# The first tile of a fused attention and two-layer kernel, cut into two units of 256 columns, with a new order for the first chunk

## The reference

```python
for t in range(S):
    kt, vt, bt = (k_n[:, :, t], v[:, :, t], beta[:, :, t, None])
    y[:, :, t] = np.einsum('bhd,bhde->bhe', q[:, :, t], state)
    v_old = np.einsum('bhde,bhd->bhe', state, kt)
    state = state + bt[:, :, :, None] * np.einsum('bhd,bhe->bhde', kt, vt - v_old)
...
h = x @ w_in                                         # layer 1, [384, 2048]
g = np.maximum(h, 0.0) + np.log1p(np.exp(-np.abs(h)))
x = g @ w_out                                        # [2048, 384]
h = x @ moe2_w_in;  g = h * np.cos(h);  out = g @ moe2_w_out
```

## Time and profile before

| | |
|---|---|
| three runs | 1145.91, 1149.58, 1151.12 us; median 1149.58 |
| profiled execution | 1146.16 us |
| its span | 1144.4 us |
| TensorE busy | 1026.4 us (90%) |
| VectorE, ScalarE, GpSimd busy | 747.3, 504.4, 328.0 us |

### The profile page before, as it was taken

One profiled execution on the slowest core, in us unless ns is written; L12 is line 12 of the kernel. 1 busy time (PEld: TensorE's weight loads), 2 busy tenths in 40 slices (PEclk: granted clock), 3 DMA queues, 4 the chain that ended last, 5 costly groups with the idle time before them and its releaser, 6 DMA issues.

```text
span 1144.4 us, 24969 instructions
## 1 busy us (share of the span) xinstructions
PE 1026.4 (90%) x10904; PEld 870.3 (76%) x10904; DVE 747.3 (65%) x1081; ACT 504.4 (44%) x802; POOL 328.0 (29%) x376
## 2 busy tenths in 40 slices
PE   3047779998999899899999999999999999999997
PEld 2046657876887787677778878889999999999996
DVE  4985444674567475837554468787777768777775
ACT  4131334355344634453463354454454545445443
POOL 3171850393069009602930017520010101001000
PEclk9556679999999999999989999999999999999999
DMA  9121301211030102011010071110202002010101
GB/s 206 49 70 30 43 1 30 47 12 43 16 57 29 28 18 43 29 29 23 9 43 16 2 221 35 60 45 1 56 1 56 1 1 56 1 28 1 29 1 28
DMA packets 101212, 42.69 MB, mean 37 GB/s; under 512 B 77008, under 2 KB 96464, under 8 KB 101104
## 3 DMA queue, kind: packets, MB, share of 16 engines
q1 hardware_dynamic: 100160, 40.90, 16.2%
q10 hardware_dynamic: 944, 0.20, 0.1%
HBM read 31.65 MB, written 9.44 MB: 36 GB/s over the span
## 4 chain that ended last, share of the span: by engine, by line
PE 63%; POOL 19%; DVE 11%; issue 4%; ACT 2%; DMA 0%; SPq 0%; DVEq 0%; ACTq 0%
POOL inv L378 10%; PE bank L1122 9%; PE bank L1124 9%; PE bank L1123 8%; POOL blk L375 8%; PE bank L1142 6%; PE bank L1144 6%; PE bank L1143 6%; DVE blk L654 3%; PE bank L1146 3%; PE bank L1148 3%; PE bank L1147 3%; PE bank L897 2%; PE bank L885 2%; PE bank L955 1%
## 5 line engine op out<-in xcount | busy, mean ns | idle before, releaser
L1122 PE MATMUL bank<-x_hi,wi_hi 128*128 128x512 f32 x576 | 236.9, 411 | 1.3 <-DVE x_lo L689 1.3
L1124 PE MATMUL bank<-x_hi,wi_lo 128*128 128x512 f32 x576 | 230.1, 399 | 0.0
L1123 PE MATMUL bank<-x_lo,wi_hi 128*128 128x512 f32 x576 | 229.5, 398 | 0.0
L580 ACT ACTIVATE tmp<-bank 128x512 f32<-128x512 f32 x96 | 57.5, 599 | 260.2 <-PE bank L1124 260.1
L839 DVE TENSOR_TENSOR g_lo<-tmp,g_hi 128x512 fp32r<-128x512 f32 x192 | 162.5, 847 | 6.6
L830 DVE SCALAR_TENSOR_TENSOR tmp<-bank,tmp 128x512 f32<-128x512 f32 x96 | 65.9, 686 | 153.7 <-ACT tmp L584 153.3
L571 ACT ACTIVATE tmp<-bank,consts 128x512 f32<-128x512 f32 x96 | 66.1, 689 | 177.2 <-PE bank L1124 177.2
L1142 PE MATMUL bank<-wo_hi,g_hi 128*128 128x384 f32 x384 | 129.5, 337 | 1.8 <-DVE g_lo L839 1.8
L1124 PEld LDWEIGHTS bank<-x_hi,wi_lo 128*128 128x128 f32 x576 | 110.2, 191 | 26.9
L1144 PE MATMUL bank<-wo_hi,g_lo 128*128 128x384 f32 x384 | 129.4, 337 | 0.0
L1143 PE MATMUL bank<-wo_lo,g_hi 128*128 128x384 f32 x384 | 129.1, 336 | 0.0
(11 more groups left out here) (100 smaller groups left out, 1572.0 us busy)
## 6 DMA issues: line engine op xcount, KB each, us to landing
stage<-in_moe_w_in SPq DMA_DIRECT2D x32, 192.0 KB, 4.4
stage<-in_moe_w_out SPq DMA_DIRECT2D x8, 768.0 KB, 5.6
kn<-in_k SPq DMA_DIRECT2D x24, 192.0 KB, 4.5
res_v<-in_v SPq DMA_DIRECT2D x24, 192.0 KB, 3.8
qn<-in_q SPq DMA_DIRECT2D x24, 192.0 KB, 4.4
x_t<-x_res SPq DMA_DIRECT2D x6, 768.0 KB, 4.2
x_raw<-x_t SPq DMA_DIRECT2D x6, 768.0 KB, 6.1
out_x<-res SPq DMA_DIRECT2D x24, 192.0 KB, 3.2
```

What stands on the lines that cost most here:

```text
L1122: mm(dst, wi_hi[:, ft, kt, :], hi[:, kt, :], start=(kt == 0), stop=False)
L1123: mm(dst, wi_hi[:, ft, kt, :], lo[:, kt, :], start=False, stop=False)
L1124: last = mm(dst, wi_lo[:, ft, kt, :], hi[:, kt, :], start=False, stop=(kt == KT - 1))
```

## The change

The first tile becomes two units of 256 columns: columns 0 to 255 are the first 64 tokens of the four batches, and need YT0 only. So there are 13 units (2, then 5 tiles of layer 1, then 6 of layer 2), and the first product is issued behind YT0 of chunk 0. In detail:

- Chunk 0's first half is written out in `begin` in an order of its own: the keys of chunk 1 are transposed and the scores P0 are computed ahead of the first substitution's end. What is left of chunk 0 (17 jobs) goes beside unit 0, chunk 1 beside unit 1, chunk c beside tile c-1.
- SLOTS is replaced by AT: for each unit the slots at which a job is issued. The first four jobs in the rows of units 2 to 5 belong to the chunk before (norms of a later chunk).
- The first substitution writes its products densely into `delta`, instead of into the unused half of `blk` with a stride.
- The norms' factors use three rows in place of four; chunk 1's keys are scaled by GpSimd. Two of the four diagonal copies of chunk 0 go to VectorE. Half of the first keys are loaded on ScalarE's queue, and the beta blocks on SP's; q and v of chunk 0 are loaded earlier; the last weight piece is loaded behind v.
- Six weight pieces instead of seven are split early by ScalarE and GpSimd; GpSimd starts the fourth once invT is set, not once `inv` is ready.

```diff
-LAST = 2 * TILES * FT
-FUSED = (TILES - 1) * FT
+
+HALF = NT // 2
+UNITS = [(0, 0, HALF), (0, HALF, HALF)] + [(t, 0, NT) for t in range(1, TILES)] + [(t, 0, NT) for t in range(TILES)]
+N1 = TILES + 1
+NU = len(UNITS)
+LAST1 = N1 * FT
+LAST = NU * FT
+FUSED = (N1 - 1) * FT
...
-FRONT = ("T0", "T1", "S0", "S1")
-ORDER = ("KS0", "M1", "Q0", "F1", "P0", "T0", "V0", "T1", "SN0", "S0", "S1", "Y0", "KS1", "V1", "YT0", "SN1",
+BEGIN = ("T0", "T1", "S0", "S1", "Q0", "P0", "+T0", "+T1", "M1", "F1", "V0", "SN0", "Y0", "YT0")
+FIRST = ("KS1", "+S0", "+S1", "V1", "Q1", "SN1", "P1", "Y1", "YT1")
+ORDER = ("KS0", "M1", "Q0", "F1", "P0", "+T0", "V0", "+T1", "SN0", "+S0", "+S1", "Y0", "KS1", "V1", "YT0", "SN1",
          "Q1", "P1", "Y1", "YT1")
...
+AT = (
+    (0, 1, 2, 3, 4, 5, 6, 7, 8, 9, 11, 12, 14, 18, 19, 20, 21),
+    (3, 7, 8, 10, 11, 12, 13, 14, 15, 16, 17, 18, 19, 20, 20, 21, 21, 22, 23, 24, 24, 25, 26, 27, 28, 29),
+    (0, 1, 2, 3, 4, 10, 11, 12, 13, 14, 15, 15, 16, 17, 18, 19, 20, 21, 21, 22, 22, 23, 24, 24, 25, 26, 27, 27, 28, 29),
...
+def jobs_at(i, slot):
+    return AT[i].count(slot)
...
         load_k(0)
         for n in range(2):
             load_piece(stage1, w1_loaded, pieces1, n)
         load_k(1)
-        for n in range(2, RING):
+        load_q(0)
+        load_piece(stage1, w1_loaded, pieces1, 2)
+        load_beta_blocks()
+        load_piece(stage1, w1_loaded, pieces1, 3)
+        load_v(0)
+        for n in range(RING, RING + 2):
+            sp.wait_ge(w_split, piece_before(n) + 1)
             load_piece(stage1, w1_loaded, pieces1, n)
-        load_v(0)
-        load_q(0)
-        for n in range(RING, NP):
+        sp.wait_ge(filled, cid(0, "Q0") + 2)
+        load_q(1)
+        for n in range(RING + 2, NP - 1):
             sp.wait_ge(w_split, piece_before(n) + 1)
             load_piece(stage1, w1_loaded, pieces1, n)
...
+        def scale_keys(c):
+            pool.wait_ge(norm_step, 6 * c + 6)
+            g = 2 * c % 4
+            keys = kn[:, g:g + 2, :, 0:D]
+            nc.gpsimd.tensor_tensor(keys, keys, norm[:, 2, :].rearrange("p (s u) -> p s u", s=2).unsqueeze(3)
+                                    .to_broadcast([P, 2, U, D]), ALU.mult).then_inc(kn_set, 1)
+
         clean(0)
-        for n in range(RING):
+        for n in range(2):
             low_weights(n)
-        pool.wait_ge(inv_ready, 1)
-        for n in range(RING, EARLY):
+        scale_keys(1)
+        low_weights(2)
+        pool.wait_ge(invT_set, 1)
+        for n in range(3, EARLY):
             low_weights(n)
         for n in range(EARLY, NP):
...
+        for s in range(2):
+            src = k[2:4].rearrange("b h s d -> s (b h) d")[s * C:(s + 1) * C, :, :]
+            nc.scalar.dma_start(kn[C:P, s, :, 0:D], src).then_inc(k_loaded[0], 16)
+        nc.scalar.dma_start(beta_rows[:, :], beta.rearrange("b h s -> (b h) s")).then_inc(beta_loaded, 16)
...
-            for n in range(RING):
+            for n in range(2):
                 high_weights(n)
+            take_transposes(0, "Q0", qT)
+            high_weights(2)
+            take_transposes(1, "T0", knT[:, fill_of(1, 0)])
+            take_transposes(1, "T1", knT[:, fill_of(1, 1)])
+            for n in range(3, EARLY):
+                high_weights(n)
+            fill_diagonal(0, (1, 0))
+            act.wait_ge(diag_set, 4)
+            take_merge(0, "M1", BLK, lambda part, s: m1[part, s], 1.0)
+            take_merge(0, "F1", 0, lambda part, s: aT[part, fill_of(0, s), :, BLK:C], -1.0)
+            take_y(0, "Y0")
+            take_x(0, 0, "YT0")
 
...
             for j in range(BLK - 1):
-                prod = blk[:, 0:j + 1, j + 1:BLK].rearrange("p c i -> p i c")
                 shape = [P, BLK - 1 - j, j + 1]
+                prod = flat(delta[:, :, :])[:, 0:shape[1] * shape[2]].rearrange("p (i c) -> p i c", c=shape[2])
...
             take_s(0, 0, "S0")
+            factors(1)
             take_s(0, 1, "S1")
             for g in range(4):
                 take_blocks(0, g)
+            take_p(0, "P0")
             first_solve()
+            turn_inverse(0)
+            dve.wait_ge(w_split, 3)
+            transpose_inverse(0)
+            dve.wait_ge(invT_set, 1)
+            for g in (3, 2):
+                rows, lo = slice(BLK * g, BLK * g + BLK), BLK * (g % 2)
+                nc.vector.tensor_copy(aT[rows, both(0), :, lo:lo + BLK],
+                                      invT[rows, :, :].rearrange("p (s u) c -> p s u c", s=2)).then_inc(diag_set, 1)
+            take_delta(0, 0, "V0")
+            take_state(0, 0, "SN0")
+            take_x(0, 0, "YT0")
 
...
                 gram(0, s)
+            pe.wait_ge(q_loaded, 32)
+            transposes(0, "Q0", qn)
+            scores(0, 0)
+            for s in range(2):
+                keys_transposed(1, s)
+            merge_inner(0)
+            merge_outer(0)
+            solve_values(0, 0, "V0")
+            add_to_state(0, 0, "SN0")
+            read_out(0, 0, "Y0")
+            turn_out(0, "YT0", "Y0")
 
...
+            t, at, w = UNITS[i]
+            if i in (0, N1):
+                await_weights(part_of(i), True, ft)
             if ft == 0:
-                if t < TILES:
-                    await_pair(pe, cid(t, "YT1"))
+                if i < N1:
+                    await_pair(pe, cid(t, "YT1" if i else "YT0"))
                 else:
-                    pe.wait_ge(x_lo_set, t - TILES + 1)
+                    pe.wait_ge(x_lo_set, t + 1)
             if before(n) is not None:
                 pe.wait_ge(h_used, before(n) + 1)
             hi, lo = x_hi[t % 2], x_lo[t % 2]
-            dst = bank[4 + ring(n)][:, :]
+            dst, cols = bank[4 + ring(n)][:, 0:w], slice(at, at + w)
             for kt in range(KT):
-                mm(dst, wi_hi[:, ft, kt, :], hi[:, kt, :], start=(kt == 0), stop=False)
-                mm(dst, wi_hi[:, ft, kt, :], lo[:, kt, :], start=False, stop=False)
-                last = mm(dst, wi_lo[:, ft, kt, :], hi[:, kt, :], start=False, stop=(kt == KT - 1))
+                mm(dst, wi_hi[:, ft, kt, :], hi[:, kt, cols], start=(kt == 0), stop=False)
+                mm(dst, wi_hi[:, ft, kt, :], lo[:, kt, cols], start=False, stop=False)
+                last = mm(dst, wi_lo[:, ft, kt, :], hi[:, kt, cols], start=False, stop=(kt == KT - 1))
...
         begin()
         jobs = attention()
-        for _ in range(JOBS):
-            next(jobs)
         product1(0)
-        for t in range(TILES - 1):
+        for i in range(N1 - 1):
             for ft in range(FT):
-                n = t * FT + ft
+                n = i * FT + ft
                 product1(n + 1)
-                for _ in range(SLOTS[2 * ft]):
+                for _ in range(jobs_at(i, 2 * ft)):
                     next(jobs)
                 product2(n)
-                for _ in range(SLOTS[2 * ft + 1]):
+                for _ in range(jobs_at(i, 2 * ft + 1)):
                     next(jobs)
...
```

More of the change, by code:

```diff
@@ L122, in build @@
         beta_blk = sb("beta_blk", [P, NCH, BLK], where=att)
-        norm = sb("norm", [P, 4, 2 * U], where=att)
+        norm = sb("norm", [P, 3, 2 * U], where=att)
         kn = sb("kn", [P, 4, U, Q2], where=att)
@@ L319, in _ @@
             load_piece(stage2, w2_loaded, pieces2, n)
-        store_x2(TILES - 2)
-        for t in (TILES, TILES + 1):
+        store_x2(N1 - 2)
+        for t in range(2):
             load_x(t)
@@ L418, in _ @@
             if n == 3:
-                low_x(TILES)
-        for t in range(TILES + 1, 2 * TILES):
+                low_x(0)
+        for t in range(1, TILES):
             low_x(t)
@@ L455, in take_merge, with fill_diagonal @@
                 last.then_inc(taken[n % 3], 1)
-        def fill_diagonal(c):
+        def fill_diagonal(c, groups):
             act.wait_ge(invT_set, c + 1)
-            for g in range(4):
+            for g in groups:
                 rows, lo = slice(BLK * g, BLK * g + BLK), BLK * (g % 2)
@@ new lines, in begin @@
+            take_delta(0, 0, "V0")
+            take_state(0, 0, "SN0")
+            take_x(0, 0, "YT0")
+        def attention():
+            take_rest(0, 1, "KS1")
+            yield
+            take_s(1, 0, "S0")
+            yield
+            take_s(1, 1, "S1")
+            yield
+            take_delta(0, 1, "V1")
+            yield
+            take_blocks(1, 0)
+            yield
+            yield
+            take_state(0, 1, "SN1")
+            yield
+            take_blocks(1, 1)
+            yield
+            take_p(0, "P1")
+            yield
+            take_blocks(1, 2)
+            yield
+            yield
+            take_blocks(1, 3)
+            yield
+            take_x(0, 1, "YT1")
+            yield
+            yield
+            reduce(2)
+            yield
+            yield
+            factors(2)
+            scale_keys(2)
+            yield
+            for c in range(1, NCH):
@@ L1039, in begin @@
                 gram(0, s)
-        def attention():
```

(39 more changed lines are left out.)

291 lines of the change are left out of this document (156 added, 135 removed), and 3 rows, old and new, of the table AT.

## The result

The changed kernel takes 1171.21 us (median of 4 runs, 1166.83 to 1173.26) against 1149.25 for the kernel before in the same pairs of runs: a ratio of 1.0187, 95% interval 1.0165 to 1.0208. It is **slower by 1.9%**, clear of noise, and outside the range of the prediction (1130 to 1159). The profiled execution took 1172.83 us.

The account below looks back on a forecast made before the run. GpSimd's substitution and the stretch from a merge to the next substitution were taken to bound the kernel. Chunk 2's substitution +1.8 us and 4.2 less behind the last merge gave -2.4: 1147 us, range 1130 to 1159.

Parts of the forecast that it names:

- Part 1: Road to the first product: copy of the merge's result at 69.6 plus 20.5 us, product at 90 instead of 131.5.
- keys loaded on two queues: Start of the front: half of the first keys on ScalarE's queue, taken to save 1.5 us.
- the dense products don't help: Rival on the first substitution: dense writing saves nothing, front 7.2 us later, +4.8, 1154 us; chance 0.10.
- Part 2: First product to chunk 1's substitution: 32.5 us, so start at 122.6 (113.75 before), merge at 175.4.
- the weight loads: Rival: weight loads bound the 256-column matmuls, 0.174 us or so each instead of 0.12, 1158 us; chance 0.15.
- it waits 8: Merge of chunk 1: TensorE could be there at about 167, merge at 175.4, so it waits 8 us.
- the ring doesn't bind: Rival: the early start is kept, less moved chunk-0 jobs and some 10 us for 256-column products, -16, 1133; chance 0.20.
- the ring: GpSimd's substitution, merge, then the stretch to the next substitution: 106.2 us per 512-token tile, taken to set the time.
- Part 3: Chunk 1's merge to chunk 2's substitution: 43.1 us instead of 53.5, so start at 218.5, 1.8 us later than before.
- Part 4: From chunk 2's substitution on: old periods kept, 4.2 us less behind the last merge, total -2.4 us.
- The sign: Whole kernel against before: chance 0.34 faster, 0.41 the same, 0.25 slower.
- the price of the split: First tile as two 256-column halves: +2 us over both units in the forecast, some 10 us in a rival.

Follow-up runs that it names:

- e5_early: Changed kernel's front and dense products, first tile whole, old slots, chunk 1's gram products and block transposes moved into the front; 1130.25 us, 0.983 of the kernel before.
- e1_odd: Changed kernel with steps from the merge (chunk 1) or the inverse's turn (chunks 2 to 4) one slot earlier, merges at odd slots; 1158.86 us, ratio 1.0068.
- e6_split: Changed kernel's front, first tile as two 256-column units, both begun after 128 tokens, slots of e1_odd from the second unit; 1167.71 us, ratio 1.0148.
- e10_halves: e5_early with its first tile as two 256-column units, both begun after 128 tokens, steps at nearly the same share of the tile; 1151.12 us, ratio 1.0008.
- e2_shift: Kernel before with all steps from the inverse's turn on one slot later, nothing else; 1181.87 us, ratio 1.0273.

## Why the prediction was wrong

**Part 1 was right.** Predicted: first product at 90, steps of 255 elements at 0.42 us, one of two VectorE copies over 3 us (they took 0.69 and 3.80). The timeline has

```profile
50.00 0.42 DVE L803 TENSOR_TENSOR delta<-blk,inv 128x255 f32<-128x255 f32 x1
...
66.33 4.52 DVE L841 COPY aT<-invT 32x1024 f32<-32x1024 f32 x2
...
66.37 3.93 POOL L427 TENSOR_TENSOR wi_lo<-stage,wi_hi 128x1536 fp32r<-128x1536 f32 x1 [33.26 <-DVE invT L820]
...
70.89 1.19 ACT L477 ACTIVATE m<-bank 32x512 f32<-32x512 f32 x2 [2.42 <-DVE aT L841]
...
92.10 0.55 PE L1284 MATMUL bank<-x_hi,wi_hi 128*128 128x256 f32 x1 [1.40 <-DVE x_lo L762]
```

The copy of `m` was due at 69.6 and came at 70.89; the product came at 92.10. A term that did not come is the 1.5 us for keys loaded on two queues: the squares start at 9.11 us, and at 8.86 in the kernel before, and the multiply ahead of the steps at 36.59 instead of 35.0. The dense steps fell from 0.59 to 0.42 us, and those of 31 elements stayed at 0.19 to 0.21, so a further element costs about 1.0 ns (0.22 us over 224 elements) where it cost 1.7: the rule of the Trainium skill named there (Vector Engine (DVE) Microarchitecture Reference, section 5.2) holds, and the rival "the dense products don't help" is out.

**Part 2 was right in its sum, and that by luck in part.** Predicted 122.6 for the substitution of chunk 1, measured 122.80: the first product was 2.1 us late, and the stretch behind it took 30.7 us for 32.5 (whose listed jobs add up to 14.9, not 14.7). Its inverse was turned after 46.5 us instead of 49.3, so the merge came at 172.85 for 175.4. The matmuls of 256 columns at full clock stand 0.12 us apart, as taken:

```profile
117.64 0.28 PE L1310 MATMUL bank<-g_lo,wo_hi 128*128 128x256 f32 x1
117.76 0.28 PE L1311 MATMUL bank<-g_hi,wo_lo 128*128 128x256 f32 x1
```

against 512 columns in e5_early

```profile
226.45 0.40 PE L1307 MATMUL bank<-g_hi,wo_lo 128*128 128x512 f32 x1
226.69 0.39 PE L1305 MATMUL bank<-g_hi,wo_hi 128*128 128x512 f32 x1
```

So the weight loads bound neither, and that rival fell. But "it waits 8" at that merge was wrong: TensorE waited 0.9, because it had already lost 10.1 us to waits for g_lo since 92. I had named this uncovered chain in the rival where the ring doesn't bind, and left it out of the forecast, since I held all work of TensorE there to be hidden by the ring.

**Part 3 was short by 6.2 us.** Predicted 43.1 us from the merge to the substitution of chunk 2, measured 49.3. In it TensorE waits 3.0 us for `m` (parity again: turn 7, transpose 8, merge 10), 1.3 for g_lo, 1.0 for delta, and the granted clock is 0.86.

**Part 4 is the step that failed:** "From here the ring has its old pieces: 53.0, then three periods, 317.2 to the last merge." Measured: 54.6 us, then 337.0. I counted how many products stand between two merges (30, 30, 31) and took their number for the whole of it. Where the steps fall within a group, which the two tables of slots give (merge at 5 before; at 12, 10 and 8 after), I did not look at: two dependent steps with a product's function between them stood in the sum at their old distance. The predicted waits of 8, 7, 6, 6 and 4 us at the merges are 0.9 and less: TensorE was never early enough. The test written into the prediction, that under 3 us each means that TensorE binds, came true, but "then the time is near 1133" did not follow, for TensorE was held up elsewhere. The 4.2 us fewer behind the last merge did not show either (557.2 for 557.5).

The account, on the profiled span (predicted 1142.0, measured 1170.9): substitution of chunk 2 +3.6, to the next merge +1.6, to the last merge +19.8, behind it +3.9, together 28.9.

**The sign.** Part 4's +19.8 was in no rival. All my slower cases were resources (loads, strides), none was the order itself. By stretch, the three periods last 339.3 us in the changed kernel, 323.1 in e1_odd and 318.7 before: 16.2 of these 20.6 us go with the one slot. In e1_odd 4.6 us are lost again ahead of them (the substitution of chunk 2 starts at 226.69 for 222.11), so 12 to 14 us arrive at the end. With its 12 us back (e1_odd, 1158.86) the kernel would have been at the upper end of the range, and still slower than the kernel before. What is left fits the second term that was mis-sized, the price of the split: 17 to 21 us in e6_split and e10_halves, which I had at 2 us in the forecast and at 10 in the rival, less the 9 to 10 us that the early start brings.

## What to carry to other kernels

Where steps are placed by hand between products, a step's place has a phase besides a distance: list, for each engine, what stands between two dependent steps before and after, for one slot later may cost what two slots later do not. Before a unit of work is halved, compare what the shorter unit of the busiest engine still covers with the latency of the chain behind it, which does not halve. And an earlier start gains only what the slowest ring lets through: here moving that ring's first input (20 us earlier, 18 us gained) was worth more than starting the products 39 us sooner.

## What the runs showed of the chip that I had not expected

- The lost time was not all waiting. The granted clock has two levels here, 1.00 and 0.50 of 2.4 GHz. In the changed kernel it is 1.00 from 267 to 282 us; TensorE then waits 5.29 us, until 286.91; from 287 to 289 the clock is 0.50, and from 291 it is 1.00 again. With several waits of 2.3 to 5.4 us in each period, its mean is 0.93 to 0.97 in the periods of the changed kernel and of e2_shift, against 0.98 to 1.00 in the kernel before, where the longest is 2.5 us. The lower clock is a third of the loss in e2_shift's periods: over three periods the busy time of the same matmuls grew by 8.1 us, and the periods by 23.8 (342.5 for 318.7).
- A VectorE pair of 32x1024 copies, SBUF to SBUF, lasted 4.52 us (66.33) beside a GpSimd weight split that ended at 70.30. The kernel before shows the same with a 128x32 multiply. It also happens in the changed kernel's period, where a function's cast, 0.43 us elsewhere, takes 1.92 us beside GpSimd's first multiply (334.20 to 336.58, above). Two of VectorE's copies gained nothing over leaving all four on ScalarE (4.30 us for four, at 279.40).

The cast, on VectorE:

```profile
334.95 1.92 DVE L962 CAST g_hi<-tmp 128x512 fp32r<-128x512 f32 x1
```
